# Where the operands of the matmuls lie in SBUF, modulo 128 bytes

## The reference

```python
scores = scale * np.matmul(q, k.transpose(0, 1, 3, 2))        # q, k, v: (2, 8, 576, 64)
Dmat = np.where(rel >= 0, gamma[:, None, None] ** rel[None, :, :], 0.0)
x = np.matmul(scores * Dmat[None], v)                          # to (1152, 512)
...
p = domain_probs / (domain_probs.sum(-1, keepdims=True) + 1e-09)
for e in range(4):                                             # w1 (512, 1024), w2 (1024, 512)
    out += p[:, e:e + 1] * (np.maximum(x @ w1[e], 0.0) @ w2[e])
...
h = x @ w_in                                                   # (512, 2048)
g = h * np.tanh(softplus(h))
return g @ w_out                                               # (2048, 512)
```

## The kernel before

| tensors | used as | bytes beyond a multiple of 128 |
|---|---|---|
| `w2_hi`, `w2_lo` | moving, layer 2 | 0 |
| `h_hi`, `h_lo` | stationary, layer 2 | 0 |
| `xa`, `xb`, `xt` | moving, layer 1 | 64 |
| `w1_hi`, `w1_lo`, `ws` | stationary, layer 1 | 64 |
| `qkv`; `ident`, `acc_sb`; `zeros` | both operands of their matmuls | 64 |
| `w_raw`, `h_act`, `part` | not of TensorE | 0 |

## Time and profile before

### The profile page before, as it was taken

How to read it: one execution, slowest core, us unless ns; L and a number is a source line. 1 busy time by engine, 2 the same in 40 slices (tenths; PEclk the granted TensorE clock), 3 DMA queues, 4 the chain that set the end, 5 groups by cost and what they waited for, 6 DMA issues and landing times.

```text
span 627.8 us, 9476 instructions
## 1 busy us (share of the span) xinstructions
PE 618.6 (99%) x3764; PEld 554.7 (88%) x3765; DVE 252.7 (40%) x388; ACT 238.2 (38%) x459; POOL 284.3 (45%) x239
## 2 busy tenths in 40 slices
PE   8899999999999999999999999999999999999997
PEld 5788899999999999999999899988988999989996
DVE  5556853323153323153323153325545432324333
ACT  3446423432223432123442223435554454344431
POOL 4557655543535542535543635532444543443300
PEclk9899999999999999999999999999999999999999
DMA  8955312322112322202322212321211233201002
GB/s 276 304 187 178 100 52 67 101 85 64 55 35 67 101 78 57 68 34 67 101 67 68 68 34 68 87 81 34 68 34 34 68 116 86 67 1 52 1 0 100
DMA packets 25146, 50.41 MB, mean 80 GB/s; under 512 B 2896, under 2 KB 3216, under 8 KB 25104
## 3 DMA queue, kind: packets, MB, share of 16 engines
q1 hardware_dynamic: 24816, 49.66, 25.8%
q10 hardware_dynamic: 288, 0.17, 0.1%
HBM read 47.45 MB, written 2.36 MB: 79 GB/s over the span
## 4 chain that ended last, share of the span: by engine, by line
PE 94%; DVE 2%; issue 1%; ACT 1%; POOL 1%; ACTq 0%; POOLq 0%
PE bank L491 29%; PE bank L493 29%; PE bank L492 29%; PE bank L445 3%; PE bank L485 2%; PE bank L623 1%; PE bank L616 1%; PE bank L449 1%; ACT h_hi L725 0%; DVE acc_sb L892 0%; DVE acc_sb L896 0%; POOL w_lo L392 0%; DVE xt L922 0%; ACT h_act L708 0%; DVE h_lo L852 0%
## 5 line engine op out<-in xcount | busy, mean ns | idle before, releaser
L392 POOL TENSOR_TENSOR w_lo<-w_raw,w_hi 128x512 fp32r<-128x512 f32 x96 | 133.2, 1400 | 152.8 <-ACT w_hi L365 152.8
L491 PE MATMUL bank<-w_hi,h_hi 128*128 128x512 f32 x432 | 168.8, 391 | 0.0
L493 PE MATMUL bank<-w_hi,h_lo 128*128 128x512 f32 x432 | 168.4, 390 | 0.0
L492 PE MATMUL bank<-w_lo,h_hi 128*128 128x512 f32 x432 | 168.3, 390 | 0.0
L387 POOL TENSOR_TENSOR ws<-ws_f,ws 128x1024 fp32r<-128x1024 f32 x24 | 57.6, 2399 | 146.4 <-ACT ws L361 146.4
L879 DVE TENSOR_TENSOR h_act<-part,bank 128x384 f32<-128x384 f32 x96 | 52.8, 550 | 162.0 <-PE bank L493 161.4
L493 PEld LDWEIGHTS bank<-w_hi,h_lo 128*128 128x128 f32 x432 | 81.1, 188 | 17.0
L492 PEld LDWEIGHTS bank<-w_lo,h_hi 128*128 128x128 f32 x432 | 81.1, 188 | 12.3
L491 PEld LDWEIGHTS bank<-w_hi,h_hi 128*128 128x128 f32 x432 | 81.0, 188 | 12.2
L730 ACT ACTIVATE part<-bank 128x384 f32<-128x384 f32 x72 | 35.4, 491 | 126.3 <-PE bank L493 126.0
L845 DVE SCALAR_TENSOR_TENSOR h_lo<-h_act,h_hi 128x384 fp32r<-128x384 f32 x64 | 55.9, 874 | 36.2 <-ACT h_hi L720 36.2
(11 more groups left out here) (87 smaller groups left out, 912.5 us busy)
## 6 DMA issues: line engine op xcount, KB each, us to landing
w_raw<-in_weights SPq DMA_DIRECT2D x144, 256.0 KB, 2.8
qkv<-in_chunks SPq DMA_DIRECT2D x18, 512.0 KB, 5.1
out<-acc_sb SPq DMA_DIRECT2D x6, 256.0 KB, 2.1
out<-acc_sb SPq DMA_DIRECT2D x1, 768.0 KB, 4.1
consts<-in_consts ACTq DMA_DIRECT2D x1, 146.0 KB, 3.8
ident<-in_consts SPq DMA_DIRECT2D x1, 64.0 KB, 4.0
consts<-in_consts SPq DMA_DIRECT2D x1, 34.0 KB, 4.0
p_nat<-in_probs ACTq DMA_DIRECT2D x1, 18.0 KB, 3.9
```

Of the source, the lines that this page charges most:

```text
L392: pool.tensor_tensor(w_lo[layer][:, x], w_raw[:, r % RAW], w_hi[layer][:, x].bitcast(F32), ALU.subtract).then_inc(s_wl, 1)
L491: pe.matmul(out, w[0], x[0], start=first, stop=False, **more)
L492: pe.matmul(out, w[0], x[1], start=False, stop=False, **more)
L493: return pe.matmul(out, w[1], x[0], start=False, stop=last, **more)
```

## The change

The high and low parts of the layer 1 tokens (`xa`, `xb`) are allocated where `h` was, and `h` where they were. Three tensors that nothing uses are put in between: `to_quarter` and `to_line`, 96 bytes a partition each, around `h`, and `to_half`, 64 bytes, ahead of `ws`. Modulo 128 bytes this gives:

| tensors | before | after |
|---|---|---|
| `w2` (moving) | 0 | 0 |
| `h` (stationary) | 0 | 32 |
| `xa`, `xb`, `xt` (moving) | 64 | 0 |
| `w1`, `ws` (stationary), `ws_f` | 64 | 64 |
| `qkv`, `xf`, `x_tmp`, `consts`, `row_decay`, `acc_sb`, `ident`, `zeros` | 64 | 0 |
| `w_raw`, `h_act`, `part` | 0 | 0 |

The order of the instructions of every engine, their shapes and their waits are the same in both kernels.

```diff
--- before.py
+++ after.py
@@ -189,8 +189,11 @@
         w2_hi = sb("w2_hi", [P, UNITS, DM], F32R)
         w2_lo = sb("w2_lo", [P, UNITS, DM], F32R)
         w_raw = sb("w_raw", [P, RAW, DM])
-        h_hi = sb("h_hi", [P, 2 * ITEMS, TC], F32R)
-        h_lo = sb("h_lo", [P, 2 * ITEMS, TC], F32R)
+
+        xa_hi = sb("xa_hi", [P, KT, TC], F32R)
+        xa_lo = sb("xa_lo", [P, KT, TC], F32R)
+        xb_hi = sb("xb_hi", [P, 3 * KH, TC], F32R)
+        xb_lo = sb("xb_lo", [P, 3 * KH, TC], F32R)
         h_act = sb("h_act", [P, 2, TC])
         part = sb("part", [P, 3, TC])
         TPP = TOKENS // P
@@ -201,11 +204,10 @@
         w1_hi = sb("w1_hi", [P, UNITS, DM], F32R)
         w1_lo = sb("w1_lo", [P, UNITS, DM], F32R)
         w_hi, w_lo = (w1_hi, w2_hi), (w1_lo, w2_lo)
-
-        xa_hi = sb("xa_hi", [P, KT, TC], F32R)
-        xa_lo = sb("xa_lo", [P, KT, TC], F32R)
-        xb_hi = sb("xb_hi", [P, 3 * KH, TC], F32R)
-        xb_lo = sb("xb_lo", [P, 3 * KH, TC], F32R)
+        sb("to_quarter", [P, 24])
+        h_hi = sb("h_hi", [P, 2 * ITEMS, TC], F32R)
+        h_lo = sb("h_lo", [P, 2 * ITEMS, TC], F32R)
+        sb("to_line", [P, 24])
         ident = sb("ident", [P, P])
         zeros = sb("zeros", [P, 512], mybir.dt.bfloat16)
 
@@ -228,6 +230,7 @@
 
         acc_sb = sb("acc_sb", [P, TPP, DM])
         xt = sb("xt", [P, 2, 4 * KH, TC], F32R)
+        sb("to_half", [P, 16])
         ws = sb("ws", [P, 2, 2, 4, KH * P], F32R)
         ws_f = sb("ws_f", [P, 4, KH * P])
 
```

## The result

The changed kernel is slower. Its median is 634.34 us (633.03 to 635.79), that of the kernel before beside it 627.93 us (626.61 to 630.64); the ratio is 1.009 with a 95% interval of 1.0062 to 1.0117, some 5.7 us.

A forecast was written before the change was run, and what follows sets the result against it. TensorE's matmul stream was taken to bound the kernel. The terms 0 - 9.7 + 0 + 0 + 0 summed to -9.7 us, giving 619.1 us from the median of 628.82 us, 1.5% faster, with a range of 600 to 634 us.

The forecast's parts named there:

- What bounds the kernel: Whole kernel: only the rate of TensorE's matmul stream can move the time by much; TensorE busy 618.6 of 627.8 us.
- (1): Moving operands of both layers: a start on a multiple of 128 alone is worth nothing, taken as 0.
- (4): VectorE, ScalarE, GpSimd and the DMA into `qkv`: their new addresses cost 0, since these engines wait for TensorE.
- (5): Attention part: 64-column matmuls and transposes keep distance 0, both operands shifting together; cost 0.
- (2): Both layers: new distance between streamed and loaded operand removes a quarter of the 38.9 us surplus, -9.7 us; chance 0.36.
- the pattern: Steps behind a change of width: 0.17, then 0.18 and 0.19 us, against 0.173 settled; taken as sign of an interaction.
- (3): Layer 2's stationary `h` at 32 modulo 128: taken as 0, bounds 0 and +8.8 us.
- this rival: `h`'s place costs: each layer 2 load makes the stream pay half the surplus again, +8.8 us, 637.6 us; chance 0.14.
- a layer 1 gain: Set against the cost of `h`'s place: 1584 x 0.0034 = 5.4 us off layer 1, giving 632.2 us.
- The rule of independent ports: Rival: weight loads take nothing from the running matmul, so addresses have no effect, 628.8 us; no effect had chance 0.34.
- The large rival: The surplus is a collision altogether that new distances avoid: up to 38.9 us off, 590 us; larger part or all, 0.16.
- the 2-byte rows: Trace rows of 2-byte matmuls on `zeros`: spacing of 0.21 us for 512 columns, used as the floor.

The follow-up runs named there:

- the shifted blocks of 512 columns: TensorE alone, blocks of 24 4-byte matmuls, moving and stationary operands both shifted by the same 32, 64 or 128 bytes: spacing as at distance 0, where it is 226.7 ns.

## Why the prediction was wrong

**What bounds the kernel** was right: TensorE's stream, and no wait of another engine in either kernel. **(1)** the moving operand's own place is worth nothing: right, and shown by the shifted blocks of 512 columns. **(4)** and **(5)**: right as far as the traces show; TensorE's waits stayed as they were, the other engines' busy times moved by under 1 us, and the first 512-column matmul did not start later.

**(2)**, the distance, is the step that failed, in its sign and in three ways: -9.7 us were forecast, and measured are -0.8 us in layer 1 and +6.8 in layer 2. First, the mechanism was right, a surplus that an interaction moves, but I took "it can move" for "it can fall": a quarter of the surplus off, 9.7 us. What the runs show is that 13.3 ns are the least of any distance tried, and that distance 0, at which both layers stood, is the one distance tried at which both widths reach it. Second, already said so: the steps that leave the settled state average 0.18 against 0.173. Departures from the settled state cost on average; one early step of 0.17 was read as a gain to be had, and the mean of the pattern, which stood in the same sentence, was not used. Third, the sentence that no row of the trace has a distance other than 0 was false. At each change of width the next layer's weights are loaded beside the other layer's stream, 64 or 192 away. The run with everything at the same place shows that these crossing distances are worth 3.9 us alone. It also shows a limit: the pattern of the earlier trace rows stands there too, at crossing distances of 0, so the pattern by itself is not the mark of a distance other than 0.

**(3)**, h at 32, was taken at 0 with an upper bound of +8.8 us, from half the surplus on each of the 1296 matmuls. Measured are 6.2 ns on each, 8.0 us in settled steps and 6.8 in all: the upper bound's size was nearly right, and that was luck. The reason given for this rival, a slice that touches one unit more, is not the cause: with both operands shifted by 32 the same slice costs nothing. The 6.2 ns are the price of distance 32, a part of (2). The case had 0.14, and the median of 634.34 us lies 0.3 us above the range. The range had cut off just the upper part of this case, since I had set a layer 1 gain against it that did not come (0.8 us of 5.4).

**The rule of independent ports** (the Trainium skill, TensorE: Matmul & The Clock Gate, "Step-by-step: what each phase is for") would have given no change. For 2-byte operands every distance gave the same 215.9 ns, as it says; for 4-byte operands the runs differ from it by up to 7.5 ns a matmul, and the measurement decides. **The large rival** rested on the 2-byte rows. No 4-byte distance came near them.

What stays open: why a 4-byte matmul costs 13.3 ns over its columns at the best distance, why fewer loaded columns cost more and not less, and what repeats every 256 bytes. The runs give the table and not the circuit.

## What to carry to other kernels

Where TensorE streams 4-byte operands without pause, put the moving and the stationary operand of a matmul at the same place modulo 256 bytes, and measure the few distances that arise where one kind of matmul follows another; here the layouts span 11 us of 628. A price that varies inside a trace is not yet a price that can be lowered: take its mean over the variation, and look for where the disputed quantity already takes other values. And a small kernel of one engine alone, with the real alternation of shapes, reproduced the full kernel's steps within a nanosecond or two and ranked 166 combinations of places in three runs.

## What the runs showed of the hardware that I had not expected

- A stream of 4-byte matmuls, each with its weight load, depends on the distance of its two operands modulo 256 bytes: 226.7 ns at 0, 228.9 at 192, 232.3 at 4 bytes and 233 to 234 at most others, for 512 columns. 2-byte operands show none of it (215.9 ns at the five distances tried).
- For 384 columns the table is another one: 173.3 ns at 0, 32, 96 and 192, and up to 176.8 at 160. At 64 and 224 it took two values in different blocks (174.7 and 176.7; 176.5 and 173.5).
- At the best distance the surplus over columns / 2.4 GHz is 13.3 ns for 512 and for 384 columns.
- Behind a change of width the steps leave their settled value for some seven matmuls, and the pattern repeats within 2 ns from stage to stage and from one program to another. It depends on the distances and on how long the stream ahead had run: the kernel before pays nothing at a change to 512 columns behind twelve of 384, and 22 ns behind six.
